# Masked attention ahead of two expert layers: alternating heads in the scores and values, a second pair of score banks, one bank for turned queries and keys

## The reference, cut to what matters

```python
# attention: q, k, v are (2, 8, 576, 64) float32
scores = scale * np.matmul(q, k.transpose(0, 1, 3, 2))
mask_local = (rel >= 0) & (rel < 32)                       # heads 0 to 3
mask_strided = (rel >= 0) & (pos[None] % 32 == pos[:, None] % 32)   # heads 4 to 7
scores = np.where(masks, scores, -1e9)
attn = exp(scores - max) / (sum + 1e-9)
x = attn @ v                                               # (2*576, 512)
# dense expert layer on x: 8 experts, 512 -> 1024 -> 512, weights by 8 rounds of row/column scaling
# then an expert layer with the two best of 8 experts for each row
```

## Time and profile before

| | |
|---|---|
| median of 3 runs | 1207.4 us (1205.65 to 1208.31) |
| the profiled execution | 1205.9 us, of which the profiled span 1204.1 us |
| mean granted clock of PE | 0.979 |
| PE busy | 1182.2 us (98%) |
| DVE, ACT, POOL busy | 488.6, 327.3, 107.0 us |
| attention with its fills | from the start to about 113 us |

### The profile page before, as it was taken

The page is one execution under the profiler, slowest core; times in us unless marked ns, Lnnn a source line. Parts: engine busy times, 40 slices in busy tenths (PEclk is TensorE's granted clock), DMA queues, the critical chain, the costliest instruction groups (busy, mean ns, idle before and its releaser), DMA issues.

```text
span 1204.1 us, 19140 instructions
## 1 busy us (share of the span) xinstructions
PE 1182.2 (98%) x6692; PEld 1053.3 (87%) x6697; DVE 488.6 (41%) x1003; ACT 327.3 (27%) x710; POOL 107.0 (9%) x118
## 2 busy tenths in 40 slices
PE   8999999999999999999999999999997999999997
PEld 5788899999999999999999999999896889888885
DVE  4645634223322421421332332251136566665663
ACT  4754113112212211311221221131131343443332
POOL 3221100000000000000000000000001222222222
PEclk9788999999999999999999999999998999999999
DMA  6623302202200400310220130040002766556653
GB/s 162 157 81 119 120 1 72 68 0 70 70 0 14 125 0 0 104 35 0 70 70 0 36 103 0 0 133 34 27 9 86 206 178 178 158 150 174 163 151 79
DMA packets 82337, 96.42 MB, mean 80 GB/s; under 512 B 22176, under 2 KB 56992, under 8 KB 82304
## 3 DMA queue, kind: packets, MB, share of 16 engines
q1 hardware_dynamic: 76400, 81.23, 22.7%
q0 software_dynamic: 5904, 14.75, 5.8%
HBM read 85.05 MB, written 10.91 MB: 80 GB/s over the span
## 4 chain that ended last, share of the span: by engine, by line
PE 96%; DVE 2%; issue 1%; DMA 0%; ACT 0%; POOLq 0%; POOL 0%; DVEq 0%
PE bank L1130 15%; PE bank L1144 15%; PE bank L1146 15%; PE bank L1145 15%; PE bank L1131 14%; PE bank L1132 14%; PE bank L1068 2%; PE bank L1100 1%; PE bank L1079 1%; PE bank L1351 1%; PE bank L1178 1%; PE bank L1273 1%; PE bank L1336 1%; PE bank L1060 1%; PE bank L1046 1%
## 5 line engine op out<-in xcount | busy, mean ns | idle before, releaser
L1144 PE MATMUL bank<-w2hi,hhi 128*128 128x512 f32 (+1 forms) x768 | 301.4, 393 | 0.0
L1146 PE MATMUL bank<-w2hi,hlo 128*128 128x512 f32 (+1 forms) x768 | 300.5, 391 | 0.0
L1145 PE MATMUL bank<-w2lo,hhi 128*128 128x512 f32 (+1 forms) x768 | 300.3, 391 | 0.0
L1130 PE MATMUL bank<-xhi,w1hi 128*128 (+1 forms) x768 | 259.1, 337 | 0.1
L1132 PE MATMUL bank<-xhi,w1lo 128*128 (+1 forms) x768 | 258.0, 336 | 0.0
L1131 PE MATMUL bank<-xlo,w1hi 128*128 (+1 forms) x768 | 257.9, 336 | 0.0
L647 ACT ACTIVATE hhi<-bank 128x384 fp32r<-128x384 f32 x184 | 90.6, 492 | 613.3 <-PE bank L1132 613.3
L745 DVE SCALAR_TENSOR_TENSOR hlo<-bank,hhi 128x384 fp32r<-128x384 f32 (+1 forms) x256 | 138.9, 543 | 267.3 <-ACT hhi L647 234.3
L1146 PEld LDWEIGHTS bank<-w2hi,hlo 128*128 128x128 f32 (+1 forms) x768 | 142.0, 185 | 33.2
L1144 PEld LDWEIGHTS bank<-w2hi,hhi 128*128 128x128 f32 (+1 forms) x768 | 142.1, 185 | 31.0
L1145 PEld LDWEIGHTS bank<-w2lo,hhi 128*128 128x128 f32 (+1 forms) x768 | 142.1, 185 | 31.1
(11 more groups left out here) (176 smaller groups left out, 885.3 us busy)
## 6 DMA issues: line engine op xcount, KB each, us to landing
w1raw<-in_moe_w_dram SPq DMA_DIRECT2D x68, 512.0 KB, 4.6
w2raw<-in_moe_w_dram SPq DMA_DIRECT2D x68, 512.0 KB, 4.3
qkraw<-in_q_dram SPq DMA_DIRECT2D x16, 144.0 KB
qkraw<-in_k_dram SPq DMA_DIRECT2D x16, 144.0 KB
out_dram<-ysb POOLq DMA_DIRECT2D x3, 768.0 KB, 7.2
x1rows<-acc SPq DMA_DIRECT2D x9, 256.0 KB, 2.0
vloc<-in_v_dram SPq DMA_DIRECT2D x8, 144.0 KB
vstr<-in_v_dram SPq DMA_DIRECT2D x8, 144.0 KB
```

Of the source, the lines that this page charges most:

```text
L1130: pe.matmul(bank[:, 0:n], wh, xh(c), start=(c == 0), stop=False)
L1144: pe.matmul(psY[tt][0:rows, :], hh, w2hi[:, f, :], start=(f == 0), stop=False)
L1145: pe.matmul(psY[tt][0:rows, :], hh, w2lo[:, f, :], start=False, stop=False)
L1146: ins = pe.matmul(psY[tt][0:rows, :], hl, w2hi[:, f, :], start=False, stop=(f == FC - 1))
```

## The change

In each unit both masks now go first, then the score matmuls of the two heads take turns tile by tile; so do the values'. The score banks of the units below 9 (`PAIRED`) alternate between 0, 1 and 4, 6; from U9 on they are 0 and 1. The second halves of queries and keys no longer have bank 6: all four turns of a pair go one after the other through bank 5 (only the first pair still has both). PE's order in a unit becomes: masks and scores, first half of the turns, transposes of both heads of U-1, second half of the turns, warming matmuls, values of U-1. `nmax` gets two buffers. The strided pairs' queries and keys are loaded with one transfer for both heads instead of two. The loops of ACT and DVE over the units keep their order.

```diff
+        PAIRED = FILL - 1
+        def pair(U):
+            return U % 2 if U < PAIRED else 0
+        def pair_before(U):
+            return U - 2 if U < PAIRED else PAIRED - 1 if U == PAIRED else U - 1
+        def psS(U):
+            return (banks[0:2], (banks[4], banks[6]))[pair(U)]
+        def psX(g, half):
+            return banks[5 + half] if g == 0 else banks[5]
...
# VectorE, maxima
-                    if U:
-                        dve.wait_ge(exp_ready, 2 * (U - 1) + h + 1)
+                    if U >= 2:
+                        dve.wait_ge(exp_ready, 2 * (U - 2) + h + 1)
...
# TensorE, transpose_half(g, n, half)
-                if n == 1:
-                    pe.wait_ge((qT_act, qT_dve)[half], g + 1)
-                elif g:
-                    pe.wait_ge(kT_ready, 2 * (g - 1) + half + 1)
+                if g == 0:
+                    if n == 1:
+                        pe.wait_ge((qT_act, qT_dve)[half], 1)
+                elif (n, half) == (0, 0):
+                    pe.wait_ge(kT_ready, 2 * g)
+                elif n == 0:
+                    pe.wait_ge(qT_act, g + 1)
+                elif half == 0:
+                    pe.wait_ge(qT_dve, g + 1)
+                else:
+                    pe.wait_ge(kT_ready, 2 * g + 1)
...
# TensorE, scores(U), both heads
+                for h in range(2):
+                    if U >= 2:
+                        pe.wait_ge(exp_ready, 2 * pair_before(U) + h + 1)
+                    elif pair(U):
+                        pe.wait_ge(kT_ready, 2)
+                    pe.matmul(by(psS(U)[h][0:rows], w, tiles * w), identb[0:rows, 0:rows], m, start=True, stop=False)
+                pe.wait_ge(qT_act, g + 1)
+                pe.wait_ge(qT_dve, g + 1)
+                pe.wait_ge(kT_ready, 2 * g + 2)
                 for t in range(tiles):
+                    for h in range(2):
...
# TensorE, values(U)
+                pe.wait_ge(pT_act, U + 1)
+                pe.wait_ge(pT_dve, U + 1)
+                if c < LOCAL_PAIRS:
                     for t in range(tiles):
+                        for h in range(2):
...
+                else:
+                    for h, t in ((0, 0), (1, 2), (0, 1), (1, 3), (1, 0), (0, 2), (1, 1), (0, 3)):
...
# TensorE, the loop over the units
-                for h in range(2):
-                    scores(U, h)
-                    if U:
-                        transpose_probs(U - 1, h)
+                scores(U)
                 if g + 1 < ALLPAIRS:
 
                     transpose_half(g + 1, U % 2, 0)
+                if U:
+                    transpose_probs(U - 1, 0)
+                    transpose_probs(U - 1, 1)
+                if g + 1 < ALLPAIRS:
                     transpose_half(g + 1, U % 2, 1)
...
-                if WARM_FROM <= U < FILL - 1:
-                    keep_warm(WARM_LOCAL if g % PAIRS < LOCAL_PAIRS else WARM_STRIDED)
+                if WARM_FROM <= U < PAIRED:
+
+                    pe.wait_ge(exp_ready, 2 * U)
+                    keep_warm(WARM_LOCAL if g % PAIRS < LOCAL_PAIRS else WARM_STRIDED, psS(U - 1)[0])
```

More of the change, by code:

```diff
@@ L159, in moe_stack_kernel @@
         pT = over("pT", [P, 2, HALF], F32)
-        nmax = over("nmax", [QT, 2, 4], F32)
+        nmax = over("nmax", [QT, 2, 2, 4], F32)
         rsum = over("rsum", [QT, 2, 4], F32)
@@ L547, in queries @@
                     act.wait_ge(scores_ready, 4 * (g - 1))
-                act.activation(T_cols(qT[g % 2], g % PAIRS, 0, half), by(psX[half], SP_ROWS), ACT.Copy,
+                act.activation(T_cols(qT[g % 2], g % PAIRS, 0, half), by(psX(g, half), SP_ROWS), ACT.Copy,
                                scale=DH ** -0.5).then_inc(qT_act, 1)
@@ L570, in exps @@
                     ins = act.activation(prs[0:rows, U % 2, h, t * w:(t + 1) * w],
-                                         psS[h][0:rows, t * w:(t + 1) * w], ACT.Exp,
-                                         bias=nmax[0:rows, h, t:t + 1], accum_out=rsum[0:rows, h, t:t + 1])
+                                         psS(U)[h][0:rows, t * w:(t + 1) * w], ACT.Exp,
+                                         bias=nmax[0:rows, U % 2, h, t:t + 1], accum_out=rsum[0:rows, h, t:t + 1])
                 ins.then_inc(exp_ready, 1)
@@ L615, in _ @@
             act.wait_ge(lgT_summed, 2)
-            act.activation(lgT1[:, 0:LT], psS[0][0:2 * E, 0:LT], ACT.Copy).then_inc(lgT_act, 1)
+            act.activation(lgT1[:, 0:LT], banks[0][0:2 * E, 0:LT], ACT.Copy).then_inc(lgT_act, 1)
             act.wait_ge(gmax_ready, 1)
@@ L715, in keys @@
                     dve.wait_ge(scores_ready, 4 * (g - 1))
-                dve.tensor_copy(T_cols(kT[g % 2], g % PAIRS, STRIDE, half), by(psX[half], SP_ROWS)
+                dve.tensor_copy(T_cols(kT[g % 2], g % PAIRS, STRIDE, half), by(psX(g, half), SP_ROWS)
                                 ).then_inc(kT_ready, 1)
@@ L761, in _ @@
                     dve.wait_ge(scores_ready, 2 * U + h + 1)
-                    if U:
-                        dve.wait_ge(exp_ready, 2 * (U - 1) + h + 1)
-                    dve.tensor_reduce(nmax[0:rows, h, 0:tiles], by(psS[h][0:rows], w, tiles * w), AX.X, ALU.max,
+                    if U >= 2:
+                        dve.wait_ge(exp_ready, 2 * (U - 2) + h + 1)
+                    dve.tensor_reduce(nmax[0:rows, U % 2, h, 0:tiles], by(psS(U)[h][0:rows], w, tiles * w), AX.X, ALU.max,
                                       negate=True).then_inc(max_ready, 1)
@@ L809, in _ @@
             dve.wait_ge(lgT_summed, 3)
-            dve.tensor_copy(lgT1[:, LT:], psS[1][0:2 * E, 0:LT]).then_inc(lgT_dve, 1)
+            dve.tensor_copy(lgT1[:, LT:], banks[1][0:2 * E, 0:LT]).then_inc(lgT_dve, 1)
             split_w2(3)
@@ L1039, in transpose_half @@
                 if half == 0:
-                    pe.wait_ge((q_in, k_in)[n][g % 2], 32 * (g // 2 + 1))
-                if n == 1:
-                    pe.wait_ge((qT_act, qT_dve)[half], g + 1)
-                elif g:
-                    pe.wait_ge(kT_ready, 2 * (g - 1) + half + 1)
+                    n_qk = sum(2 if j % PAIRS < LOCAL_PAIRS else 1 for j in range(g % 2, g + 1, 2))
+                    pe.wait_ge((q_in, k_in)[n][g % 2], 16 * n_qk)
+                if g == 0:
[9 more added lines that the diff above has]
+                    pe.wait_ge(kT_ready, 2 * g + 1)
@@ L1045, in transpose_half, with scores @@
                 for t in range(4):
-                    ins = pe.transpose(psX[half][:, t * SP_ROWS:(t + 1) * SP_ROWS],
+                    ins = pe.transpose(psX(g, half)[:, t * SP_ROWS:(t + 1) * SP_ROWS],
                                        qkraw[g % 2][:, n, (4 * half + t) * P:(4 * half + t + 1) * P], ident[0:SP_ROWS, 0:SP_ROWS])
                 ins.then_inc(qk_transposed, 1)
-            def scores(U, h):
+            def scores(U):
                 g, c, half = U // 2, (U // 2) % PAIRS, U % 2
@@ L1061, in scores @@
-                for t in range(tiles):
[L1062 to L1070, removed]
@@ new lines, in scores @@
+                pe.wait_ge(qT_dve, g + 1)
+                pe.wait_ge(kT_ready, 2 * g + 2)
+                for t in range(tiles):
+                    for h in range(2):
+                        if c < LOCAL_PAIRS:
+                            key = query = (half * tiles + t) * rows
+                        else:
+                            head, step, _ = strided_tile(half, h, t)
+                            query = (head * SP_T + step) // 2 * rows
+                            key = STRIDE + query
+                        ins = pe.matmul(psS(U)[h][0:rows, t * w:(t + 1) * w],
+                                        qT[g % 2][h * DH:(h + 1) * DH, query:query + rows],
+                                        kT[g % 2][h * DH:(h + 1) * DH, key:key + w],
+                                        start=False, stop=(t == tiles - 1))
+                        if t == tiles - 1:
+                            ins.then_inc(scores_ready, 1)
@@ L1091, in values @@
                     pe.wait_ge(v_in[g % 2], 16 * n_v)
-                for h in range(2):
-                    pe.wait_ge((pT_act, pT_dve)[h], U + 1)
+                pe.wait_ge(pT_act, U + 1)
+                pe.wait_ge(pT_dve, U + 1)
+                if c < LOCAL_PAIRS:
                     for t in range(tiles):
[L1095 to L1100, removed]
+                        for h in range(2):
+                            ins = pe.matmul(psO[h * DH:(h + 1) * DH, t * rows:(t + 1) * rows],
+                                            vloc[g % 2][:, h, half * tiles + t, :],
+                                            pT[0:w, h, t * rows:(t + 1) * rows], start=True, stop=True)
+                else:
+                    for h, t in ((0, 0), (1, 2), (0, 1), (1, 3), (1, 0), (0, 2), (1, 1), (0, 3)):
+                        head, step, to = strided_tile(half, h, t)
+                        ins = pe.matmul(psO[head * DH:(head + 1) * DH, to * rows:(to + 1) * rows],
```

(11 more changed lines are left out.)

30 lines of the change are left out of this document (11 added, 19 removed).

## The result

The changed kernel takes 1245.5 us (median of 4 runs, 1244.1 to 1246.3), the kernel before 1206.5 (median of its 4): 1.035 times as long, 95% interval 1.030 to 1.040. The profiled execution took 1244.1 us, of which the span is 1242.3, 38.2 us more than the 1204.1 of before. The forecast was 1243, with a range of 1215 to 1256.

A forecast was written before the change was run, and what follows sets the result against it. The prediction took attention to be bound by PE's queue and its clock. Terms 28.5 + 5.6 + 2.4 = 36.5 us on the profiled 1205.9 gave 1242.4; the median, 1.5 higher, gave 1243 to 1244, range 1215 to 1256.

The forecast's parts named there:

- The wait, its place and its order in the queues: Before second turns, PE waits for bank 5: ACT's queries copy in even units, DVE's keys in odd; about 2.1 to 5.0 us.
- The longer chain: Attention units at full clock lengthen by the wait on copies; an even local unit takes 5.9 us, against 4.55.
- 3.3 + 5.6: With full clock everywhere, U10 starts 3.3 us later and U10 to U13 take 5.6 us more.
- Half clock from U1 to U9: PE at 1.2 GHz from U1 or U2 to U9's logits: 79.3 us, U10 28.5 later; chance 0.51.
- rival C: Clock falls only in the strided units, from U4: 22 us instead of 28.5, about 1236 us; chance 0.24.
- I add 2.4 for one or two: Allowance in U10 to U13: a unit meeting half clock pays about 1.8 us; 2.4 for one or two.
- units with fill: U10 to U13, which turn a next pair from one pair of score banks: together 5.6 us more on 26.9.
- rival D: Clock falls in nearly every one of U10 to U13 too: 8 to 10 us more, about 1252; chance 0.07.
- Full overlap of the scores: In score blocks, the two heads' alternating matmuls overlap fully: saving 0.86 us per local unit, 0.73 per strided.
- the local values: Values matmuls of local units: twelve in 1.0 us become pairs taking 0.6; bounds 0 and 0.5 saved.
- A: PE's queue stays the bound in attention and packing is all profit: 16.7 us less, 1190; chance 0.04.
- B: The clock never falls in attention: 3.3 + 5.6, so 1215 to 1217 us; chance 0.12.

The follow-up runs named there:

- the kernel with warming: The changed kernel plus eight matmuls of 512 columns before the second turns of U1 to U13: 1216.0 us, ratio 1.014 to the kernel before.
- the early copies: The changed kernel with only the four copies of turned queries and keys moved forward in ACT's and DVE's queues: 1197.9 us, ratio 0.998 to the kernel before.
- the packed kernel: Changed kernel with two turn banks and one score-bank pair again, plus more warming matmuls from U1 to U8: 1189.8 us, ratio 0.990 to the kernel before.
- packing alone: The changed kernel with two banks for the turns and one pair of score banks again: 1197.3 us, ratio 0.996 to the kernel before.

## Why the prediction was right

**The wait, its place and its order in the queues** were as forecast. It was read from the program: a copy that frees a bank stands behind the exponentials in ACT's list, and PE reaches the matmul that needs the bank long before. U2's first exponential came 2.35 us after its first mask (2.36 forecast), the second turns 4.87 after (5.0).

**The longer chain.** The term 3.3 + 5.6 = 8.9 us, which like the forecast compares with a kernel before that has its half-clock stretch, measured as 9.5 to 11 in all where warming held the clock (1216.0 against 1206.5 of the first comparison, 1204.8 of its own). Its parts were less exact than the whole. U1 began at 17.3 for the 16.25 walked, because U0's six warming matmuls stood at half clock (2.77 us in the changed kernel's trace); U1 to U9 were 1.4 longer than walked, U10 to U13 1.9, of which U10 has 1.1, with 3.4 us at half clock in it. Behind U13 the kernel with warming was 2.1 shorter than the kernel before, where the prediction had nothing.

**Half clock from U1 to U9.** Forecast 79.3 us and U10 at 96.6; measured 75.8 and 93.1. U1 and most of U2 still had full clock, and so had 3.4 us at U5 (mean of the stretch 0.59, of U5 0.72 in the row below). That lies between the forecast and rival C. A unit's half-clock length was right where it was wholly at 0.50: U6 9.6 for 9.8, U8 8.96 for 9.0; the furthest off was U3, 8.1 for 7.6.

```profile
46.97:54.77 7.80, 5.59 (x55) 3.66 (x53) 4.09 (x11) 4.15 (x19) 0.98 (x2) 0.72 0.60 187
```

Here 2.4 GHz came back in the dense logits of U9 (at 92.5) and at every fill that ran at half clock, near its end or at most 1.1 us behind it. It also came back at 17.4, behind six warming matmuls, and at 48.1, behind three and a unit's ordinary work. Of the eight waits for queries or keys that began at full clock six saw it fall; U1's of 2.25 us and U10's of 2.62 us did not.
The Trainium skill says ("TensorE: Matmul & The Clock Gate", "What's actually happening") that the throttled clock is the default and activity releases it. The logits and fills agree, but being busy was not enough: U8 of the kernel before stayed at 0.50 with PE busy for 7.70 of 7.70 us.

**The term that was mis-sized: "I add 2.4 for one or two"** units with fill. All four fell to half clock, U11 to U13 in the wait before the second turns, U10 (at 99.3) in the wait for `pT` behind them. Each then stayed there for 6.8 us, through nearly its whole fill; U11 from 109.5 to 116.4. Its second turns take 0.74 us for 0.47, behind the wait:

```profile
109.80 0.74 PE L1070 MATMUL bank<-ident,qkraw 72*128 72x72 f32 x4 [2.06 <-DVE kT L732]
```

U10 to U13 took 43.6 us for the 34.4 of the same chain in the kernel with warming in the wait, so 9.2 instead of 2.4. This was rival D's mechanism and its price of 8 to 10, with a chance of 0.07. With it, the kernel lost 16.8 there instead of 8.0. Behind U13 it gained 3.5 against before, which the prediction set at nothing. Of that 1.9 lie before the second layer: before had half clock in U14 and in U15 (3.4 us each, for U14), the changed kernel once there, from 140 us. The other 1.6 lie in the expert layers, where before stood 13.6 us at half clock (from 864 to 932) and the changed kernel 10.2 (from 953 to 970). The total came within 2.5 us because these errors (about -3.6, +8.8 and -3.5) nearly cancel, and not because each term was good to that: this part was luck.

Small slips of the sums change nothing: the nine units at half clock add to 79.4 (79.3 written), an even strided unit to 6.6 (6.5), and U12, 6.27 us in the kernel before, grows by 1.6 on its way to 7.9, not by 1.35.

**Packing.** Full overlap of the scores, taken from the nearest row, was right: twelve take 0.90 where six took 0.89. For the local values the walk took 0.6 us for 1.0, a saving of 0.4; the row, at full clock, has 0.72 for 1.08, a saving of 0.36:

```profile
22.20 0.72 PE L1126 MATMUL bank<-pT,vloc 128*64 128x96 f32 x12
```

What no part of the sum asked was how much of the overlap needs turns at all.
The Trainium skill ("TensorEngine Tiling (Array Packing)", "PSUM Bottleneck") warns that tiling does not speed up the emptying of PSUM, which may become the bottleneck. The 18.1 + 14.8 us of waits in the changed kernel are for copies that empty bank 5, but their place in the queues makes them late, as the early copies show, and not the tiling. In the packed kernel at full clock the warning explains 1.1 us, the waits for the exponentials that read the score banks; the 1.8 for GpSimd's scaling are no emptying of PSUM.

**Rivals.** A fell by 14.8 + 18.1 us of waits. B would have been right for a kernel that keeps its clock: its 1215 to 1217 is what was measured with the warming matmuls, 1216, with the parts off as said above. C was nearer to where the clock fell (at 27.6, with U1 and U2 mostly at full clock) than the forecast's U1, yet U3 was already at half. D came true in the units with fill.

## What to carry to other kernels

When two buffers become one, look up where in its engine's list the instruction stands that empties the buffer: in an in-order queue its place, not its 0.4 us, is the price: moving four copies took 1245.5 us to 1197.9 with the one bank kept. A wait of TensorE can be paid twice, once as a longer chain and again as everything that runs at half clock behind it. Here the first was 21 us and the second 29, and matmuls that compute nothing bought the second back. When the kernel before loses its clock in some runs, compare at like granted clock as well: otherwise the longer chain seems to cost 9.5 us here. Put small matmuls for different halves of the array next to each other first, and let them take turns only then.

## What the runs showed of the hardware that was not expected

Score blocks of two heads issued one after the other, six instructions for rows 0 to 63 and then six for rows 64 to 127, overlap without taking turns. In windows of about 0.025 us on line 1095 of the kernel without alternation the matmuls in flight go up by two near 102.46, one 6 ns behind the other. One head's instructions alone start 0.11 us apart.

```profile
102.34:102.37 0.03, 0.03 (x2) 0.03 (x2) 1.00 0.00 0
102.45:102.48 0.03, 0.03 (x4) 0.03 (x3) 1.00 0.00 0
```

The block takes 1.12 us instead of 1.64 where the two are parted. Which head's instruction started there the rows don't tell; that it was the second head's first, ahead of the rest of the first head's, is argued from the spacing and not shown.

And the fall of the clock is no function of the idle alone. In packing alone PE waited 0.85 us at the longest from U1 to the fall at 41.5, and then stood at half clock for 23.9 us, as the kernel before did from 44.8. In the profiled run of packing with 26 warming matmuls more, about 0.2 us each at full clock, it stayed at 1.00 from 16.3 us, in U1, to the end of attention. Nor is the fall the same in every run of one program: two of the ten runs of packing alone had a mean clock of 0.990 and took 1191.6 us, the others 0.976 to 0.980 and 1196.4 to 1199.4.
